# Three edits at the head of a fused attention and MLP kernel: an earlier gate, another PSUM bank, zeroed rows

## The chip, the cores and the metric

One core of a Trainium2 chip. The metric is the device time of one execution in microseconds, as the median of several.

## The reference

A gated linear attention, followed by two MLPs on its output. B=4, H=8, S=768, D=48.

```python
for t in range(S):                       # per batch and head
    cur = einsum('bhd,bhe->bhde', u * k[t], v[t])
    y[t] = einsum('bhd,bhde->bhe', r[t], state + cur)
    state = w[t][..., None] * state + einsum('bhd,bhe->bhde', k[t], v[t])
x = y.transpose(0, 2, 1, 3).reshape(3072, 384)
h = x @ w_in                             # 384 x 2048
x = (h * clip(h + 3, 0, 6) / 6) @ w_out  # 2048 x 384
out = ((x @ w1) * (x @ w2) @ w3) @ w_out2   # 384 x 1024, 1024 x 1024, 1024 x 384
```

All of it is float32.

## The kernel before

**Attention.** The 3072 tokens are cut into 12 groups (`p`) of 256, each of two chunks (`g` = 2p, 2p+1), each of two halves of 64 tokens. Arrays by row (`r_sb`, `k_sb`, `w_sb`) hold two heads: one in rows 0 to 47, one in rows 64 to 111. Rows 48 to 63 belong to no head. The tiles have 112 rows, and every VectorE operation on them and the transpose by TensorE go over all 112. The first of the two loads of each tile takes 64 rows of the source, so that rows 48 to 63 get finite values which are never used; the second takes 48 rows. Per group VectorE scales k and r by products of decays (`scale(p, n)`, n = 0 to 5), TensorE multiplies them at four levels (`level_products`), the products are merged into `A_own` (levels 0 and 1 by VectorE, levels 2 and 3 by ScalarE), and then come a transpose of k (TURN), the new states (STATES), and two steps READ_A and READ_B, each with a product of `A_own` and v (`read`) and one of state and r (`read_states`). `y_copy` then takes y out of PSUM. `scale(p, n)` for n of 2 or more waits for the products of level n-2. Four products by token per chunk, which need tokens loaded once more in another layout (`tok_a`, `tok_b`), are made by GpSimd and summed by VectorE (`sum_bands`); the load of the next such tokens waits for a sum.

**MLPs.** The first is cut into 96 slots of 128x512 hidden values: `hidden(n)` on TensorE, `clip(n)` on ScalarE, `gate(n)` on VectorE, then `split_gated(n)` (ScalarE) and `rest_of_gated(n)` (VectorE), which split the result into two fp32r parts, then `project(n)` on TensorE. Each matmul of float32 is three passes over such parts. The weights come in 16 pieces (0 to 7 of `w_in`, 8 to 15 of `w_out`), each loaded into a stage, rounded by ScalarE and its remainder formed by VectorE (both named `split_weight(q)`, L594 and L993). The stages are memory that `gated`, `g_hi` and `g_lo` use later; pieces 6 and 7 lie where `g_lo[0]` will be. Pieces 6 to 11 are issued by SyncE after the attention output has been moved into `x_sb`, piece q only when an earlier piece in its stage is split. `form_w34` forms w3 times w_out2 on TensorE; its 16 half steps stand between the attention steps of groups 0 and 1.

**Order.** Each engine's order is written out by hand for groups 0 and 1; from slot 0 on, a loop over the slots places the steps of the next groups among them. Before the first data TensorE runs eight matmuls of `y_sb`, twice recorded each, that compute nothing (`keep_busy`); they wait for the memset of `y_sb`. TensorE before: attention(1, 0), form_w34(4, 0), READ_B of group 0, form_w34(4, 1), its `read_states`, form_w34(5, 0), attention(1, 1), ... In `level_products`, level 1 of group 1 waits for `y_out` 2, since level 1 writes both banks of `ps_lv`, of which `y_bank` gives bank 1 to y. The loads of SyncE stand in the order of its `_` function: w, k, r of group 0, the first weights, tokens, v, w, k, r of group 1, and so on.

Of the kernel before, what the change touches and what calls it, by code (L numbers as in the profile page):

```python
# [11 lines left out]
B, H, S, D = 4, 8, 768, 48  # L12
# [4 lines left out]
HB = 64  # L17
# [84 lines left out]
def gated_linear_attention_two_mlps(nc, rT, kT, wT, r, k, v, w, u, w_in, w_out, w1, w2, w3T, w_out2,  # L102
# [3 lines left out]
    with ctx:  # L106
# [14 lines left out]
        def sem(name):  # L121
            return ctx.enter_context(nc.semaphore(name))
# [84 lines left out]
        y_zeroed = sem("y_zeroed")  # L207
        d_loaded = [sem(f"d_loaded{i}") for i in range(2)]
# [109 lines left out]
        def y_bank(half):  # L318

            return ps_lv[:, 1, :] if half else ps_att  # L320
# [38 lines left out]
        def _(sp):  # L359
            def load_by_row(dst, src, p, loaded):  # L360

                b, s0 = p * GT // S, p * GT % S
                for row, first, count in ((0, 0, HB), (HB, D, D)):
                    sp.dma_start(dst[row:row + count, :, :],  # L364
                                 src[first:first + count, b, :, s0:s0 + GT]
                                 ).then_inc(loaded[p % 2], 16)

            def load_w(p):
                load_by_row(w_sb, wT, p, d_loaded)

            def load_k(p):
                load_by_row(k_sb[p % 2], kT, p, d_loaded)

            def load_r(p):
                load_by_row(r_sb[p % 2], rT, p, r_loaded)
# [216 lines left out]
        def _(act):  # L592
# [33 lines left out]
            def y_copy(g):  # L626
                act.wait_ge(y_done, g + 1)
                if g >= 2:
                    act.wait_ge(x_moved[g % 2], CHUNK_X * (g // 2))
                y = y_sb[g % 2][:].rearrange("d a (half t) -> d half a t", t=SUB)  # L630
                of_half = [y_bank(half)[:, 0:PAIRS * SUB].rearrange("d (a t) -> d a t", t=SUB)
                           for half in range(2)]
                copy(y[:, 0], of_half[0][0:HP])
                for h in range(2):
                    last = copy(y[h * HB:h * HB + D, 1], of_half[1][y_row(1, h):y_row(1, h) + D])
                last.then_inc(y_out, 1)
# [101 lines left out]
            split_weight(3)  # L738
            store_w34(5)
            merge(1, 2)  # L740
# [4 lines left out]
            split_x(1)  # L745
            merge(1, 3)
            store_w34(7)
            split_weight(6)
            split_weight(7)
            act.wait_ge(three_made, 1)  # L750
            act.wait_ge(w_lo_done, 2)
            clip(0)
            split_weight(8)
# [58 lines left out]
        def _(dve):  # L812
# [203 lines left out]
            def rest_of_gated(n):  # L1016
                dve.wait_ge(g_hi_done, n + 1)
                if n >= 2:
                    dve.wait_ge(x2_part, n - 1)
# [3 lines left out]

            nc.vector.memset(three[:], 3.0).then_inc(three_made, 1)
# [30 lines left out]
            merge(1, 0)  # L1055
            split_weight(0)
            split_weight(1)
            scale(1, 3)
            merge(1, 1)
            sum_bands(2)  # L1060
            split_weight(2)
            scale(1, 4)
            split_weight(3)
            sum_bands(3)
# [3 lines left out]
            scale(1, 5)  # L1068
            keep(4)
            start(2)  # L1070
            start(3)
            split_weight(5)
            split_weight(6)
            split_weight(7)
            gate(0)
# [40 lines left out]
        def _(pe):  # L1116
# [8 lines left out]
            def level_products(p, step):  # L1125
# [7 lines left out]
                elif p == 1 and step == 1:  # L1133
                    pe.wait_ge(y_out, 2)
# [53 lines left out]
            def read(g):  # L1188
# [8 lines left out]
                for a in range(PAIRS):  # L1197
                    for half in range(2):
                        rows = slice(half * SUB, (half + 1) * SUB)
                        for h in range(2):  # L1200
                            first, at_row = c * DM + (2 * a + h) * D, y_row(half, h)
                            last = nc.tensor.matmul(
                                y_bank(half)[at_row:at_row + D, y_cols(a)],
# [5 lines left out]
            def read_states(g):  # L1209
# [6 lines left out]
                for a in range(PAIRS):  # L1216
                    for n in taking:
                        at_col = cols_of(p, c, a).start + n % 2 * SUB
                        for h in range(2):
                            rows, at_row = slice(h * HB, h * HB + D), y_row(n % 2, h)  # L1220
                            last = nc.tensor.matmul(
                                y_bank(n % 2)[at_row:at_row + D, y_cols(a)], state[n % 4][rows, a, :],
# [34 lines left out]
            def project(n):  # L1257
# [4 lines left out]
                if i == 0 and t > 0:  # L1262
                    pe.wait_ge(x2_copied, t)
# [53 lines left out]
            attention(0, READ_B)  # L1317
            form_w34(4, 1)
            attention_rest(0, READ_B)
            form_w34(5, 0)  # L1320
            attention(1, 1)
            form_w34(5, 1)
            form_w34(6, 0)
            attention(1, 2)
            form_w34(6, 1)
            attention(1, 3)
# [114 lines left out]
```

## Time and profile before

| | us |
|---|---|
| median of 3 runs | 898.12 (897.38 to 900.26) |
| the profiled execution | 897.8 |
| its span, first to last instruction | 896.0 |
| TensorE matmul busy | 878.5 |
| VectorE busy | 531.1 |
| ScalarE busy | 327.5 |
| GpSimd busy | 220.9 |

The profile is of one execution. Times of rows count from the span's start. Busy time of TensorE is of overlapping matmuls, so a busy TensorE isn't one at its peak; an idle one is idle. "PEld" is its weight load, "SPq" a queue's issue of a transfer. L594, L814 and L993 are helper lines, used by many operations: the tile names tell them apart.

### The profile page before, as it was taken

How to read it: one execution, taken by the hardware profiler on the slowest of the kernel's cores; microseconds unless marked ns; L12 is line 12 of the kernel's file. 1: busy time of each engine (PE TensorE's matmuls, PEld its weight loads, DVE VectorE, ACT ScalarE, POOL GpSimd, SP SyncE). 2: the span in 40 equal slices, each digit the busy share in tenths (PEclk: the TensorE clock that was granted, in tenths of full speed). 3: DMA queues.
4: the chain of work that ended last, by engine and by line, in shares of the span. 5: the costliest groups of instructions: out<-in, count | busy, mean ns of one | idle time of the engine just before them, and what ended most of it. 6: DMA issues, size and time to landing. Idle time of an engine off the chain costs nothing.

```text
span 896.0 us, 23934 instructions
## 1 busy us (share of the span) xinstructions
PE 878.5 (98%) x10452; PEld 790.8 (88%) x10452; DVE 531.1 (59%) x765; ACT 327.5 (37%) x556; POOL 220.9 (25%) x200
## 2 busy tenths in 40 slices
PE   8989899999999999999999999999999999999998
PEld 4557899999999999999999999998888888888887
DVE  4888997788887878786878734633231222323121
ACT  0435453435353535343444444632221312222212
POOL 0374245445444544444535000000000000000000
PEclk9998999999999999999999999999999999999999
DMA  9987653525252525353443102530010202010001
GB/s 289 339 262 240 203 136 105 155 89 162 82 161 81 160 83 159 92 150 99 144 129 92 37 21 79 181 112 1 12 60 1 71 0 71 1 36 1 25 11 36
DMA packets 62646, 93.31 MB, mean 104 GB/s; under 512 B 8215, under 2 KB 48622, under 8 KB 62542
## 3 DMA queue, kind: packets, MB, share of 16 engines
q1 hardware_dynamic: 59934, 88.36, 32.4%
q10 hardware_dynamic: 2608, 3.43, 1.3%
q8 instruction: 82, 1.34, 0.7%
q14 instruction: 22, 0.18, 0.1%
HBM read 76.03 MB, written 11.01 MB: 97 GB/s over the span
## 4 chain that ended last, share of the span: by engine, by line
PE 81%; DVE 8%; SPq 4%; DMA 3%; issue 2%; ACT 1%; ACTq 0%; DVEq 0%
PE ps_acc L1118 11%; PE ps_acc L1119 10%; PE ps_acc L1120 10%; PE ps_h L1118 10%; PE ps_h L1120 10%; PE ps_h L1119 10%; PE ps_lv L1119 4%; PE ps_lv L1120 4%; PE ps_lv L1118 4%; PE ps_lv L1152 3%; SPq L415 3%; DMA w3T_sb<-in_w3T 2%; DVE r_sb L814 1%; DVE k_sb L814 1%; SPq L364 1%
## 5 line engine op out<-in xcount | busy, mean ns | idle before, releaser
L550 POOL TENSOR_TENSOR tok_a<-tok_a 128x384 f32<-128x384 f32 x120 | 153.2, 1303 | 185.3 <-DMA tok_a<-in_k 185.3
L1118 PE MATMUL ps_acc<-g_hi,w_out_hi 128*128 128x256 f32 x576 | 169.9, 295 | 0.0
L1118 PE MATMUL ps_h<-x_hi,w_in_hi 128*128 128x256 f32 x576 | 165.3, 287 | 1.9 <-DVE gated L1012 1.9
L1119 PE MATMUL ps_h<-x_hi,w_in_lo 128*128 128x256 f32 x576 | 162.5, 282 | 0.0
L1120 PE MATMUL ps_h<-x_lo,w_in_hi 128*128 128x256 f32 x576 | 162.2, 282 | 0.0
L1119 PE MATMUL ps_acc<-g_hi,w_out_lo 128*128 128x256 f32 x576 | 162.0, 281 | 0.0
L1120 PE MATMUL ps_acc<-g_lo,w_out_hi 128*128 128x256 f32 x576 | 161.5, 280 | 0.0
L594 ACT ACTIVATE g_hi<-gated 128x512 fp32r<-128x512 f32 x144 | 90.9, 632 | 166.7 <-DVE gated L1100 107.8
L1100 DVE TENSOR_TENSOR gated<-gated,ps_lv 128x512 f32<-128x512 f32 x48 | 33.1, 689 | 186.3 <-PE ps_lv L1120 186.3
L1118 PEld LDWEIGHTS ps_h<-x_hi,w_in_hi 128*128 128x128 f32 x576 | 109.2, 190 | 4.1 <-DVE w_in_lo L993 2.0
L1118 PEld LDWEIGHTS ps_acc<-g_hi,w_out_hi 128*128 128x128 f32 x576 | 108.4, 188 | 4.0
L1119 PEld LDWEIGHTS ps_h<-x_hi,w_in_lo 128*128 128x128 f32 x576 | 109.3, 190 | 0.1
L1120 PEld LDWEIGHTS ps_h<-x_lo,w_in_hi 128*128 128x128 f32 x576 | 109.3, 190 | 0.0
L1120 PEld LDWEIGHTS ps_acc<-g_lo,w_out_hi 128*128 128x128 f32 x576 | 108.7, 189 | 0.0
L1119 PEld LDWEIGHTS ps_acc<-g_hi,w_out_lo 128*128 128x128 f32 x576 | 108.4, 188 | 0.0
L1020 DVE TENSOR_TENSOR g_lo<-gated,g_hi 128x512 fp32r<-128x512 f32 x96 | 76.0, 792 | 44.1 <-ACT g_hi L594 44.1
L692 ACT ACTIVATE gated<-ps_h,three 128x512 f32<-128x512 f32 x96 | 65.9, 686 | 71.4 <-PE ps_h L1120 71.3
L1012 DVE SCALAR_TENSOR_TENSOR gated<-gated,ps_h 128x512 f32<-128x512 f32 x96 | 65.6, 683 | 36.2 <-ACT gated L692 36.2
L594 ACT ACTIVATE gated<-ps_h 128x512 f32<-128x512 f32 x48 | 28.7, 598 | 109.8 <-PE ps_h L1120 109.8
L1120 PE MATMUL ps_acc<-w_lo,g_hi 128*128 128x384 f32 x192 | 64.6, 336 | 0.0
L1119 PE MATMUL ps_acc<-w_hi,g_lo 128*128 128x384 f32 x192 | 64.4, 336 | 0.0
L1118 PE MATMUL ps_acc<-w_hi,g_hi 128*128 128x384 f32 x192 | 64.3, 335 | 0.0
(97 smaller groups left out, 1541.5 us busy)
## 6 DMA issues: line engine op xcount, KB each, us to landing
tok_a<-in_r SPq DMA_DIRECT2D x21, 768.0 KB
tok_a<-in_w SPq DMA_DIRECT2D x21, 384.0 KB
v_sb<-in_v SPq DMA_DIRECT2D x12, 384.0 KB, 3.7
x_scratch<-x_out SPq DMA_DIRECT2D x12, 384.0 KB, 4.3
x_in<-x_scratch SPq DMA_DIRECT2D x6, 768.0 KB, 5.7
tok_a<-in_k SPq DMA_DIRECT2D x22, 192.0 KB
out<-x_out SPq DMA_DIRECT2D x5, 768.0 KB, 4.0
x_sb<-y_sb SPq DMA_DIRECT2D x144, 24.0 KB, 1.8
```

Of the source, the lines that this page charges most:

```text
L415: sp.dma_start(x_sb[g % 2][row % P:row % P + n, row // P, :], y_sb[g % 2][at_row:at_row + n, head // 2, :]).then_inc(x_moved[g % 2], 16)
L550: return nc.gpsimd.tensor_tensor(dst, x, y, ALU.mult)
L594: return nc.scalar.activation(dst, src, ACT.Copy, **scale)
L692: nc.scalar.activation(gated[n % 2][:], ps_h[n % 2][:], ACT.Relu, bias=three[:]).then_inc(relu_done, 1)
L814: return nc.vector.tensor_tensor(dst, x, y, ALU.mult)
L1012: nc.vector.scalar_tensor_tensor(out=gated[n % 2][:], in0=gated[n % 2][:], scalar=6.0, in1=ps_h[n % 2][:], op0=ALU.min, op1=ALU.mult).then ...
L1020: nc.vector.tensor_tensor(g_lo[n % 2][:], gated[n % 2][:], g_hi[n % 2][:].bitcast(F32), ALU.subtract).then_inc(g_lo_done, 1)
L1100: nc.vector.tensor_tensor(gated[n % 2][:], gated[n % 2][:], ps_lv[:, n % 2, :], ALU.mult).then_inc(ab_made, 1)
L1118: nc.tensor.matmul(psum, hi, moving_hi, start=start, stop=False)
L1119: nc.tensor.matmul(psum, lo, moving_hi, start=False, stop=False)
L1120: return nc.tensor.matmul(psum, hi, moving_lo, start=False, stop=stop)
L1152: last = nc.tensor.matmul(psum[s0:s0 + count, h, first:first + SUB // 2] .rearrange("s (n l) -> s n l", l=size), k_g[rows, s:s + count], of_r,
```

## The change

Three edits.

1. `y_bank(p, half)`: for group 0, half 1 of y goes to bank 2 of `ps_acc`, no longer to bank 1 of `ps_lv`. Hence level 1 of group 1 has no wait for `y_out`, and `project(0)` gets one (it writes `ps_acc`). TensorE runs levels 1, 2 and 3 of group 1 earlier by one to three half steps of `form_w34`; VectorE runs `scale(1, 3)` and `merge(1, 1)` ahead of the first two remainders of `w_in`, and its later scalings earlier too. `sum_bands(3)` and the splits of x come after `scale(1, 5)`.
2. `gate(0)` on VectorE stands ahead of the remainders of pieces 6 and 7, and `clip(0)` on ScalarE ahead of their roundings. `rest_of_gated(0)` waits for the remainders, whose stages it writes.
3. Rows 48 to 63 are no longer loaded. VectorE writes zeros to rows 32 to 63 of five tiles by five memsets, ahead of its other two memsets; the loads of rows 0 to 47 of groups 0 and 1 wait for them and come after those of rows 64 to 111.

```diff
-        def y_bank(half):
-            return ps_lv[:, 1, :] if half else ps_att
+        def y_bank(p, half):
+            if half == 0:
+                return ps_att
+            return ps_lv[:, 1, :] if p else ps_acc[:, KT - 1, :]
...
-                for row, first, count in ((0, 0, HB), (HB, D, D)):
-                    sp.dma_start(dst[row:row + count, :, :],
-                                 src[first:first + count, b, :, s0:s0 + GT]
+                for h in (1, 0):
+                    if h == 0 and p < 2:
+                        sp.wait_ge(rows_zeroed, zeroed_at)
+                    sp.dma_start(dst[h * HB:h * HB + D, :, :],
+                                 src[h * D:(h + 1) * D, b, :, s0:s0 + GT]
                                  ).then_inc(loaded[p % 2], 16)
...  ScalarE
             split_weight(3)
+            merge(1, 2)
             store_w34(5)
-            merge(1, 2)
             split_weight(4)
             store_w34(6)
             split_weight(5)
             split_x(0)
             split_x(1)
+            store_w34(7)
             merge(1, 3)
-            store_w34(7)
-            split_weight(6)
-            split_weight(7)
             act.wait_ge(three_made, 1)
             act.wait_ge(w_lo_done, 2)
             clip(0)
+            split_weight(6)
+            split_weight(7)
             split_weight(8)
...  VectorE
             def rest_of_gated(n):
                 dve.wait_ge(g_hi_done, n + 1)
+                if n == 0:
+                    dve.wait_ge(w_lo_done, NP)
...
+            for unused in (w_sb, k_sb[0], r_sb[0], k_sb[1], r_sb[1]):
+                nc.vector.memset(unused[HB // 2:HB, :, :], 0.0).then_inc(rows_zeroed, 1)
             nc.vector.memset(three[:], 3.0).then_inc(three_made, 1)
             nc.vector.memset(y_sb[0][:], 0.0).then_inc(y_zeroed, 1)
...
             merge(1, 0)
+            scale(1, 3)
+            merge(1, 1)
             split_weight(0)
             split_weight(1)
-            scale(1, 3)
-            merge(1, 1)
+            scale(1, 4)
             sum_bands(2)
             split_weight(2)
-            scale(1, 4)
             split_weight(3)
+            scale(1, 5)
+            keep(4)
             sum_bands(3)
             split_x(0)
             split_x(1)
             split_weight(4)
-            scale(1, 5)
-            keep(4)
             start(2)
             start(3)
             split_weight(5)
+            gate(0)
             split_weight(6)
             split_weight(7)
-            gate(0)
             split_weight(8)
...  TensorE
-                elif p == 1 and step == 1:
-                    pe.wait_ge(y_out, 2)
...  project(n)
-                if i == 0 and t > 0:
+                if n == 0:
+                    pe.wait_ge(y_out, 2)
+                elif i == 0:
                     pe.wait_ge(x2_copied, t)
...
             attention(0, READ_B)
+            attention(1, 1)
             form_w34(4, 1)
             attention_rest(0, READ_B)
             form_w34(5, 0)
-            attention(1, 1)
+            attention(1, 2)
             form_w34(5, 1)
+            attention(1, 3)
             form_w34(6, 0)
-            attention(1, 2)
             form_w34(6, 1)
-            attention(1, 3)
             form_w34(7, 0)
             form_w34(7, 1)
```

## Rows read from the trace of the kernel before

**Rows 1.** The page: span and busy times of the engines.
```profile
span 896.0 us, 23934 instructions
PE 878.5 (98%) x10452; PEld 790.8 (88%) x10452; DVE 531.1 (59%) x765; ACT 327.5 (37%) x556; POOL 220.9 (25%) x200
```

**Rows 2.** Windows: length, busy time (count) by engine, TensorE's granted clock, DMA share, GB/s.
```profile
73.00:75.00 2.00, 2.00 (x12) 1.47 (x11) 2.00 (x6) 0.18 (x1) 0.16 (x1) 1.00 1.06 398
...
140.00:160.00 20.00, 20.00 (x356) 19.04 (x355) 16.39 (x22) 6.79 (x13) 11.37 (x12) 1.00 0.27 89
```

**Rows 3.** The chain that ended last, in order of time: start, us, what.
```profile
77.82 3.05 DVE w_in_lo L993 x2
...
121.85 0.61 DVE r_sb L814
122.51 0.76 PE ps_lv L1152 x50
```

**Rows 4.** Who waited for whom, VectorE, 40 to 135 us: total, times, longest.
```profile
DVE totals L814 <- PE ps_lv L1152: 3.4, 1, 3.4
DVE w_in_lo L993 <- ACT w_in_hi L594: 2.3, 1, 2.3
```

**Rows 5.** Timeline, 0 to 13 us: start, us, engine, line, what [idle before].
```profile
0.81 0.06 DVE L1024 MEMSET three<- 128x1 f32 x1 [0.81 <-PEq L1430]
0.86 0.96 POOL L545 MEMSET A_own<- 128x1024 f32 x1
0.95 0.48 DVE L1025 MEMSET y_sb<- 112x512 f32 x1
1.49 6.32 PE L1278 MATMUL ps_acc<-y_sb 112*128 112x512 f32 x8 [1.49 <-DVE y_sb L1025]
7.64 1.88 PE L1278 MATMUL ps_lv<-y_sb 112*128 112x512 f32 x4
12.05 1.08 PE L1152 MATMUL ps_acc<-r_sb,k_sb 48*60 48x32 f32 x64 [0.81 <-DVE r_sb L814]
```

**Rows 6.** Timeline of TensorE, 43 to 74 us.
```profile
43.41 1.08 PE L1152 MATMUL ps_acc<-r_sb,k_sb 48*60 48x32 f32 x64 [1.03 <-DVE r_sb L814]
45.11 2.85 PE L1289 MATMUL ps_h<-w_out_sb,w3T_sb 128*128 128x384 f32 x8 [0.62 <-DMA w3T_sb<-in_w3T]
66.63 0.76 PE L1152 MATMUL ps_lv<-r_sb,k_sb 48*32 48x32 f32 x64 [1.98 <-DVE r_sb L814]
73.98 0.57 PE L1118 MATMUL ps_h<-x_hi,w_in_hi 128*128 128x256 f32 x1
```

**Rows 7.** Timeline of VectorE and GpSimd, 34 to 58 us.
```profile
34.36 4.78 POOL L550 TENSOR_TENSOR tok_b<-tok_b 128x384 f32<-128x384 f32 x4
35.37 1.51 DVE L814 TENSOR_TENSOR totals<-w_sb 112x512 f32<-112x512 f32 x1 [0.85 <-DMA k_sb<-in_kT]
...
48.95 2.67 POOL L550 TENSOR_TENSOR tok_a<-tok_a 128x384 f32<-128x384 f32 x2 [9.80 <-DMA tok_a<-in_k]
49.32 3.11 DVE L993 TENSOR_TENSOR w_in_lo<-w_stage,w_in_hi 128x768 fp32r<-128x768 f32 x2
56.17 1.50 DVE L814 TENSOR_TENSOR k_sb<-k_sb,totals 112x512 f32<-112x512 f32 x1
```

**Rows 8.** Timeline of VectorE, 74 to 84 us.
```profile
74.60 0.95 DVE L993 TENSOR_TENSOR w_in_lo<-w_stage,w_in_hi 128x768 fp32r<-128x768 f32 x1
80.79 0.67 DVE L1012 SCALAR_TENSOR_TENSOR gated<-gated,ps_h 128x512 f32<-128x512 f32 x1
82.47 1.49 DVE L1020 TENSOR_TENSOR g_lo<-gated,g_hi 128x512 fp32r<-128x512 f32 x1
```

**Rows 9.** Timeline of ScalarE, 74 to 79 us: pieces 6 and 7 of w_in.
```profile
76.93 1.59 ACT L594 ACTIVATE w_in_hi<-w_stage 128x768 fp32r<-128x768 f32 x2 [0.40 <-DMA w_stage<-in_w_in]
```

**Rows 10.** Timeline of SyncE's queue, 45 to 69 us.
```profile
45.05 0.33 SPq L385 DMA_DIRECT2D tok_b<-in_r  x1
67.88 1.06 SPq L404 DMA_DIRECT2D w_stage<-in_w_in  x2
```

More of the change, by code:

```diff
@@ L207, in gated_linear_attention_two_mlps @@
         y_zeroed = sem("y_zeroed")
+        rows_zeroed = sem("rows_zeroed")
         d_loaded = [sem(f"d_loaded{i}") for i in range(2)]
@@ L359, in _, with load_by_row @@
         def _(sp):
-            def load_by_row(dst, src, p, loaded):
+            def load_by_row(dst, src, p, loaded, zeroed_at):
                 b, s0 = p * GT // S, p * GT % S
-                for row, first, count in ((0, 0, HB), (HB, D, D)):
-                    sp.dma_start(dst[row:row + count, :, :],
-                                 src[first:first + count, b, :, s0:s0 + GT]
+                for h in (1, 0):
[3 more added lines that the diff above has]
+                                 src[h * D:(h + 1) * D, b, :, s0:s0 + GT]
                                  ).then_inc(loaded[p % 2], 16)
             def load_w(p):
-                load_by_row(w_sb, wT, p, d_loaded)
+                load_by_row(w_sb, wT, p, d_loaded, 1)
             def load_k(p):
-                load_by_row(k_sb[p % 2], kT, p, d_loaded)
+                load_by_row(k_sb[p % 2], kT, p, d_loaded, 2 + 2 * (p % 2))
             def load_r(p):
-                load_by_row(r_sb[p % 2], rT, p, r_loaded)
+                load_by_row(r_sb[p % 2], rT, p, r_loaded, 3 + 2 * (p % 2))
             def load_tok(g):
@@ L630, in y_copy @@
                 y = y_sb[g % 2][:].rearrange("d a (half t) -> d half a t", t=SUB)
-                of_half = [y_bank(half)[:, 0:PAIRS * SUB].rearrange("d (a t) -> d a t", t=SUB)
+                of_half = [y_bank(g // 2, half)[:, 0:PAIRS * SUB].rearrange("d (a t) -> d a t", t=SUB)
                            for half in range(2)]
@@ L1202, in read @@
                             last = nc.tensor.matmul(
-                                y_bank(half)[at_row:at_row + D, y_cols(a)],
+                                y_bank(p, half)[at_row:at_row + D, y_cols(a)],
                                 v_sb[rows, first:first + D], A_own[rows, h, c, a, :],
@@ L1221, in read_states @@
                             last = nc.tensor.matmul(
-                                y_bank(n % 2)[at_row:at_row + D, y_cols(a)], state[n % 4][rows, a, :],
+                                y_bank(p, n % 2)[at_row:at_row + D, y_cols(a)], state[n % 4][rows, a, :],
                                 flat(r_sb[p % 2])[rows, at_col:at_col + SUB],
```

## The prediction

> **What bounds the kernel now.** I read the busy times and the windows first, then the chain that ended last, then the waits of VectorE, then the timelines of the places that these name. TensorE is busy 878.5 of 896.0 us [rows 1], and in a window such as that from 140 us it has no idle time while VectorE has 3.6 us in 20 [rows 2]: there the kernel is paced by TensorE, and nothing in this change touches it. The chain shows another picture of the head. From about 55 us to 121.85 it runs through VectorE nearly all the way; the last piece of it is a scaling, 0.61 us from 121.85, which lets TensorE start a level product at 122.51 [rows 3]. So the end moves by as much as VectorE's list moves at that handover. On that list VectorE has, from 40 us on, two waits of over 0.5 us ahead of the handover: 3.4 us for level 1 of group 1 and 2.3 us for piece 6 of w_in [rows 4]. So at most 5.7 us can be had, 0.6% of the time, and the question is whether the time that is won at the first wait is kept at the second. Before 45 us the chain isn't VectorE's: a load of w3T holds TensorE until 45.11 [rows 6].
>
> **Edit 1, the bank.** Level 1 of group 1 no longer waits for y and comes right behind READ_B's first part. With nothing else changed, VectorE would find its products at about 49.5, have 0.2 us of wait for them where it had 3.4, and run ahead by some 3 us. The order of the rest costs nothing by itself: the same operations, and GpSimd's product pass from 48.95 lies beside whichever stands there. A scaling pass of 512 columns takes 1.50 us beside it [rows 7], and 0.6 on the chain where GpSimd is idle [rows 3]; the two remainders that change places with it are slowed likewise (3.11 us for two [rows 7], 0.95 for one without GpSimd [rows 8]). I price this exchange at 0, with 0.8 us to either side, one pass caught or missed.
>
> **Edit 3, at the start.** Five memsets of 1024 columns now stand ahead of that of y_sb on VectorE's queue, and TensorE's dummy matmuls wait for y_sb. The memset of 512 columns takes 0.48 us and that of one column 0.06 [rows 5]: 0.82 ns for each further column, 0.90 us for 1024, 4.5 us for five. Bounds: 2.4 us if 1024 columns cost no more than 512 (5 x 0.48), 4.8 us by GpSimd's memset of 1024 columns (5 x 0.96) [rows 5]. So the dummies start at 6.0 and not at 1.49.
>
> The Trainium skill (VectorE: DVE Perf Modes, "Zero memsets can be issued as uint32") says that a memset takes one cycle per element; at the 0.96 GHz it gives for VectorE that would be 1.07 us each, an estimate of 5.3 us for five, and 0.8 us more of late start. The row of 512 columns speaks against it slightly: by the rule it would take 0.53 us, the trace has 0.48.
>
> The dummies are 16 records. Eight take 6.32 us, the next four 1.88 [rows 5]: the first run at the lower of TensorE's two clock levels (0.86 us each, 1.2 GHz), and the change to 0.43 us each (2.4 GHz) comes some 5.2 us after the first. All of them take from 1.49 to 11.24, 9.7 us, and the first level product then waits 0.81 us for VectorE and starts at 12.05 [rows 5]. If the clock rises as long after the start as before, the dummies end at 6.0 + 9.7 = 15.7, less the overlap of the last two, and the level product starts at about 15.5: 3.5 us late. If it rose at the same moment as before, it would be 1.3 us; if 1.5 us later, with the dearest memsets, 5 us. I take 3.5, because the rise follows work.
>
> The wait for memsets in SyncE's queue: the first load of rows 0 to 47 waits from 1.4 to about 1.8 us and the next ones less. The loads and issues behind them come 0.3 us later, and each is 14% smaller (96 rows for 112). k_sb lands at 8.2, which TensorE, busy until 15.5, doesn't see. What is saved up to 45 us is six loads of 16 rows of 4 KB, 0.39 MB, at the 398 GB/s of a full DMA stream [rows 2] 1.0 us: w3T lands at about 44.
>
> **Where the late start goes.** TensorE runs without a gap from 12.05 to 42.38. Then it has two waits: 1.03 us for a scaling until 43.41 and 0.62 us for w3T until 45.11 [rows 6]. A scaling 1.1 us later (below) and w3T 1 us earlier leave both covered: TensorE uses 1.65 us of slack and is 3.5 - 1.65 = 1.85 us late at READ_B, 49.7 for 47.89. What is late next is VectorE: update(0) waits for the states, 3.5 us late, so scale(1, 0) starts at 37.9 for 35.37; GpSimd ends its pass at 39.1 (34.36 + 4.78) [rows 7], so two of the three operations cost 0.6 for 1.5 us, and VectorE is 1.1 us late at sum_bands(1). On that sum waits SyncE's queue: the token loads at 45.05 [rows 10] come 1.1 us late and with them all 20 transfers of x and everything behind them.
>
> **The list from 50 us, with both.** READ_B's first part ends at 50.3; merge(1, 0) to 51.2; level 1 at 50.3 to 51.4; scale(1, 3) beside GpSimd 3.3 us, to 54.7; merge(1, 1) 0.6; two remainders 2.7; VectorE is at 58.0, where before it had done the same by 59.6 (56.17, two passes of 1.50 and a merge of 0.6, less overlaps [rows 7]). That is 1.6 us ahead, what is left of 3.4 after 1.85. Level 2 comes at 57.5 (three half steps of 2.75 us behind 51.4 less the reads), its scaling at 58.6 to 61.8, sum_bands(2) 2.7, remainders 2 and 3 2.2, scale(1, 5) 1.4, keep 0.3, sum_bands(3) 2.4, x 0.9, piece 4 0.9, start 1.4, piece 5 0.9: 74.9 for 75.5 [rows 8].
>
> **Edit 2, the gate.** gate(0) (0.67 us [rows 8]) needs hidden(0). TensorE now has four half steps of w34 behind level 3, at 62.5: 4 x 2.75 = 11.0, so hidden(0) runs from 73.5 to 75.9 (before: a gap of 1.98 us, level 3 from 66.63, and only two half steps, which took until 73.98, 6.6 us, longer than 5.5 as they ran partly at the lower clock [rows 6]). clip(0) ends at 76.7, gate(0) at 77.3. It lies in what is still VectorE's wait for piece 6 and takes 0.6 us off the list behind it. Piece 6: its rounding starts at 76.93, held by the transfer [rows 9], which was issued at 67.88 [rows 10] into a stream that is full (398 GB/s from 73 to 75 us [rows 2]). The issue is 1.1 us later; k and r of group 2 are 0.13 MB smaller, 0.35 us. It lands at 76.9 + 1.1 - 0.35 = 77.7, or up to 0.4 us sooner, as piece 8 is issued later. The remainder of piece 6 then starts at 78.3, 0.5 us later than before (77.82 [rows 3]), behind its rounding of 0.8 (1.59 us for two [rows 9]). Pieces 6 and 7 take 3.05 [rows 3], piece 8 1.1: rest_of_gated(0) starts at 82.4 for 82.47 [rows 8]. Sum: +0.5 (piece 6) - 0.6 (the gate moved) = -0.1 us. The added waits cost nothing: y_out 2 is signalled at about 56, w_lo_done 8 one operation ahead on the same engine. From 82.5 to 122.4 VectorE has no wait and its list is the same, so this shift arrives. TensorE's wait of 1.9 us before slot 2 vanishes, but TensorE isn't what ends last there; nor do smaller loads later matter, with the DMA share at 0.27 [rows 2].
>
> 897.8 - 0.1 = 897.7 for the profiled execution; the median of the runs shown is 0.3 above it: 898.0.
>
> **The rivals.** (a) Part of it is kept. If the start costs 1.3 us only, TensorE's slack takes all of it, SyncE isn't late, piece 6 lands at 76.5, its remainder starts at 77.4 and the gate is out of the way: -0.4 - 0.6 = -1.0, 897.1. For it: the clock could rise at a time that isn't tied to the first dummy. Against: the row that shows 5.2 us. Chance 0.22. (b) Faster beyond the measurement. If piece 6 is there when VectorE asks for it, at 75.5 less what is gained, the whole of both waits is had: its remainder at 75.0, the gate behind it hidden, -2.8 to -3.5 us, 895.0. For it: 0.5 MB fewer bytes ahead of it and piece 8 no longer beside it. Against: the stream is full [rows 2] and 0.13 MB is 0.35 us of it. Chance 0.12. (c) The late start is felt in part. 5 us at the start leave 3.4 at READ_B and 2.6 on SyncE's queue; piece 6's remainder at 79.8: +2.0 - 0.6 = +1.4, 899.4. Chance 0.16. (d) Slower beyond it: the late start reaches SyncE's queue whole, since update(0), 3.5 to 5 us late, holds scale(1, 0) and GpSimd's pass still slows it. Then token loads, x moves and piece 6 are 3.5 to 4 us late, the remainder of piece 6 starts at 81.3, +3.5 - 0.6 = +2.9: 901.0. It decides from where sum_bands(1) is over 3.6 us late. Against: GpSimd's pass ends at 39.1, and VectorE had 0.85 us of wait there for k [rows 7]. Chance 0.08. (e) The change doesn't do what it says: level 1 comes no sooner than now, as y's other bank is held. Nothing on bank 2 of ps_acc is waited for after the merge of level 2 of group 0, so I put this under (c).
>
> **How the numbers follow.** The forecast, 898.0, has 0.42. A difference of 0.3%, 2.7 us, is about what a measurement of this kernel tells from none; the forecast, (a) and (c) lie within it. Same 0.80, faster 0.12, slower 0.08. The range leaves out the tails of (b) and (d): from 895.8, between (a) and (b), to 900.2, between (c) and (d).
>
> **What would show it.** In the new profile: the dummies starting near 6.0 and the first level product near 15.5 (edit 3 priced right); waits of TensorE at 42 to 45 us gone; level 1 of group 1 near 50.3, and no wait of 3.4 us on VectorE; SyncE's token loads near 46; piece 6's rounding held by its transfer at 77.3 to 77.7, with gate(0) ahead of it; rest_of_gated(0) near 82.4; the last VectorE hold on TensorE near 122.4. It is wrong if TensorE's start isn't late, if piece 6 lands before 76 or after 79, or if VectorE gets a wait between 82 and 122.

## The result, and the profile after

The changed kernel takes 908.02 us (906.78 to 909.24, 4 runs) where the kernel before takes 898.59 (897.38 to 900.26, 4 runs): ratio 1.0099, interval 1.0084 to 1.0115. It is slower by 9.4 us; the forecast was 898.0, no change. The profiled execution took 906.78 us with a span of 905.0, against 897.8 and 896.0 before [rows 1].

The page after, span and busy times, to read beside [rows 1]:

```profile
span 905.0 us, 23940 instructions
...
PE 878.6 (97%) x10452; PEld 792.2 (88%) x10452; DVE 541.7 (60%) x770; ACT 328.1 (36%) x556; POOL 223.4 (25%) x200
```

TensorE's busy time is the same to 0.1 us, so the 9 us are idle time of TensorE. VectorE's is 10.6 us more; five memsets of 0.91 explain 4.6 of them. The rest is other operations that took longer.

The timeline of VectorE after, from 0 to 7 us, answers to [rows 5]:

```profile
1.01 0.91 DVE L1032 MEMSET w_sb<- 32x1024 f32 x1 [1.01 <-PEq L1439]
2.08 0.91 DVE L1032 MEMSET k_sb<- 32x1024 f32 x1 [0.16 <-issue]
...
6.39 0.48 DVE L1034 MEMSET y_sb<- 112x512 f32 x1
```

And that of TensorE:

```profile
6.93 6.22 PE L1287 MATMUL ps_acc<-y_sb 112*128 112x512 f32 x8 [6.93 <-DVE y_sb L1034]
12.99 1.88 PE L1287 MATMUL ps_lv<-y_sb 112*128 112x512 f32 x4
...
16.51 1.08 PE L1159 MATMUL ps_acc<-r_sb,k_sb 48*60 48x32 f32 x64
```

Each memset has a busy time of 0.91 us, as forecast, but the next starts 1.07 us after it. The dummies start 5.44 us later than before and the first level product 4.46 later (12.05 to 16.51), since the wait of 0.81 us before it is gone and the dummies took 0.1 less (16.58 - 6.93 for 11.24 - 1.49).

The timeline of VectorE after, from 44 us, a stretch of which the prediction said that the order of the rest costs nothing:

```profile
48.21 2.08 DVE L911 COPY_PREDICATED A_own<-diag,corner 128x256 f32<-128x256 uint8 x2
50.19 1.15 DVE L958 TENSOR_TENSOR state<-kept,added 112x192 f32<-112x192 f32 x1
51.26 1.08 DVE L819 TENSOR_TENSOR totals<-totals 112x128 f32<-112x128 f32 x1
52.26 1.48 DVE L819 TENSOR_TENSOR k_sb<-k_sb,totals 112x512 f32<-112x512 f32 x1
53.66 1.48 DVE L819 TENSOR_TENSOR r_sb<-r_sb,totals 112x512 f32<-112x512 f32 x1
55.06 0.69 DVE L931 COPY_PREDICATED A_own<-lmask,ps_acc 124x512 f32<-124x512 uint8 x1
```

The same operations in the kernel before, VectorE, from 45.88 us:

```profile
45.88 0.78 DVE L906 COPY_PREDICATED A_own<-diag,corner 128x256 f32<-128x256 uint8 x2
46.56 0.35 DVE L953 TENSOR_TENSOR state<-kept,added 112x192 f32<-112x192 f32 x1
46.83 0.28 DVE L814 TENSOR_TENSOR totals<-totals 112x128 f32<-112x128 f32 x1
47.03 0.68 DVE L814 TENSOR_TENSOR k_sb<-k_sb,totals 112x512 f32<-112x512 f32 x1
47.63 0.68 DVE L814 TENSOR_TENSOR r_sb<-r_sb,totals 112x512 f32<-112x512 f32 x1
```

GpSimd after, the pass for chunk 2, which began at 48.95 before [rows 7]:

```profile
47.85 2.14 POOL L555 TENSOR_TENSOR tok_a<-tok_a 128x384 f32<-128x384 f32 x2 [8.02 <-DMA tok_a<-in_k]
```

Before, start(1), update(3) and scale(1, 2), the first five rows of each list, were done at 48.31, 0.64 us ahead of the pass. After, they come 2.33 us later and the pass 1.1 us sooner; start(1) begins 0.36 us behind the start of the pass, and all five rows lie in it (its last row ends at 56.0). They take 6.93 us, start of the first to end of the last, where they took 2.43: 4.5 us more. merge(1, 0), the sixth row, takes 0.69 us in the pass as it did outside; its data come from PSUM (`ps_acc`).

Who waited for that is seen in the timeline of TensorE after, from 43 us (before: [rows 6]):

```profile
43.48 2.85 PE L1298 MATMUL ps_h<-w_out_sb,w3T_sb 128*128 128x384 f32 x8
...
50.47 0.67 PE L1209 MATMUL ps_acc<-A_own,v_sb 64*48 64x64 f32 x32
55.89 1.34 PE L1159 MATMUL ps_lv<-r_sb,k_sb 48*56 48x32 f32 x64 [4.76 <-DVE A_own L931]
57.16 4.15 PE L1298 MATMUL ps_h<-w_out_sb,w3T_sb 128*128 128x384 f32 x8
61.24 0.67 PE L1228 MATMUL ps_acc<-r_sb,state 48*48 48x64 f32 x32
```

The two waits of before at 42 to 45 us are gone. But level 1 of group 1 waits 4.76 us, for merge(1, 0) (L931). The diff takes away the branch of p = 1 and step = 1, so level 1 falls into the general one below it:

```python
                elif step > 0:
                    pe.wait_ge(merged[p % 2], level(p, step - 1))
```

A wait for merge(1, 0) has thus taken the place of the wait for y_out. It is only the last part of the 4.76 us: level 1 also waits for scale(1, 2), which ends at 55.14, 4.0 us after TensorE was free (51.14); merge(1, 0) ends 0.6 us after that. Behind level 1 on TensorE stand form_w34(4, 1), which takes 4.15 us for 2.85 (the granted clock is 0.60 from 56 to 58 us and 0.54 from 58 to 60, so most of it ran at the lower of the two levels, 1.2 GHz; the engine had stood idle for the 4.76 us before), and then the second part of READ_B, `read_states`, at 61.24. Before, it came at 51.26. It gives y, which ScalarE copies (y_copy(1), 62.24 for 52.29), and y goes through SyncE's queue, which waits 6.8 us for it; in the list of its waits before there is none for y. SyncE after (before: [rows 10]):

```profile
49.69 20.49 SPq L420 DMA_DIRECT2D x_sb<-y_sb  x20
...
74.31 0.99 SPq L409 DMA_DIRECT2D w_stage<-in_w_in  x2
```

Pieces 6 and 7 are issued at 74.31 for 67.88. VectorE after, where they are used (before: [rows 8]):

```profile
82.80 0.69 DVE L1017 SCALAR_TENSOR_TENSOR gated<-gated,ps_h 128x512 f32<-128x512 f32 x1 [2.10 <-ACT gated L697]
85.27 2.68 DVE L998 TENSOR_TENSOR w_in_lo<-w_stage,w_in_hi 128x768 fp32r<-128x768 f32 x2 [1.78 <-ACT w_in_hi L599]
...
89.55 1.48 DVE L1027 TENSOR_TENSOR g_lo<-gated,g_hi 128x512 fp32r<-128x512 f32 x1
```

The chain that ended last, after (before: [rows 3]):

```profile
55.14 0.62 DVE A_own L931
55.89 1.34 PE ps_lv L1159 x63
57.23 4.09 PE ps_h L1298 x8
...
66.52 1.11 SPq L420
...
74.86 10.59 DMA w_stage<-in_w_in
85.47 0.86 ACT w_in_hi L599
86.35 1.60 DVE w_in_lo L998
...
130.31 0.76 PE ps_lv L1159 x50
```

rest_of_gated(0) is 7.1 us late (89.55 for 82.47) and the level product that the chain hangs on is 7.8 us late (130.31 for 122.51). The last 1.2 of the span's 9.0 us come later; this section doesn't place them.

### The profile page after: what moved, and what is told of

Same layout as the page of the kernel before. It is cut to its first block, busy times and chain, and to the rows that moved or that the text cites. A ratio compares the mean times of both kernels' runs of the same rounds, so it can differ in the third digit from the quotient of the medians.

```text
span 905.0 us, 23940 instructions
## 1 busy us (share of the span) xinstructions
PE 878.6 (97%) x10452; PEld 792.2 (88%) x10452; DVE 541.7 (60%) x770; ACT 328.1 (36%) x556; POOL 223.4 (25%) x200
## 4 chain that ended last, share of the span: by engine, by line
PE 78%; DVE 9%; SPq 6%; issue 3%; DMA 2%; ACT 1%; DVEq 0%; ACTq 0%
PE ps_acc L1127 11%; PE ps_acc L1128 9%; PE ps_acc L1129 9%; PE ps_h L1127 9%; PE ps_h L1129 9%; PE ps_h L1128 9%; SPq L420 5%; PE ps_lv L1128 4%; PE ps_lv L1129 4%; PE ps_lv L1127 4%; PE ps_lv L1159 3%; PE ps_h L1298 2%; DVE k_sb L819 2%; DVE r_sb L819 2%; DMA w_stage<-in_w_in 1%
## 5 line engine op out<-in xcount | busy, mean ns | idle before, releaser
L555 POOL TENSOR_TENSOR tok_a<-tok_a 128x384 f32<-128x384 f32 x120 | 150.6, 1282 | 192.7 <-DMA tok_a<-in_k 192.7
```

Of the source, the lines that this page charges most:

```text
L555: return nc.gpsimd.tensor_tensor(dst, x, y, ALU.mult)
```

## The experiments

The kernel before, run beside the experiments, took 899.41 us (31 runs) for the first four in the order of the text, 898.54 (28) for the next four, and 899.46 (35) for the last four. By the ratios the loss of the changed kernel is 8.9 us. Each kernel of the table ran ten times, but the changed one four, "y ahead of level 1" seven and the last two twelve times; each profile is of one execution, whose time is given where it isn't near the median. The expectations name theories by letter. **A**: the late start (edit 3) pushes VectorE's start(1), update(3) and scale(1, 2) into GpSimd's pass for chunk 2, and edit 1 has put y behind level 1, which waits for them. The rivals: **B**, the new order costs by itself; **C**, edit 3 costs by itself; **D**, it is the smaller loads or their waits; **E**, the contention acts through VectorE's list, and not through y being held; **F**, the pass isn't what slows VectorE; **G**, the added wait for merge(1, 0) is most of the loss; **H**, whatever is gained before 77 us ends in the wait for piece 6.

| kernel | median (lowest to highest) | ratio to before, interval |
|---|---|---|
| changed kernel | 908.02 (906.78 to 909.24) | 1.0099, 1.0084 to 1.0115 |
| edit 1 alone | 898.78 (897.14 to 901.02) | 0.9996, 0.9984 to 1.0009 |
| edit 2 alone | 900.28 (898.84 to 901.82) | 1.0007, 0.9994 to 1.0019 |
| edit 3 alone | 900.68 (899.14 to 902.31) | 1.0015, 1.0004 to 1.0026 |
| edits 1 and 2 | 899.80 (897.70 to 904.43) | 1.0007, 0.9988 to 1.0025 |
| y_sb's memset first | 898.30 (897.03 to 900.35) | 0.9993, 0.9980 to 1.0006 |
| y_sb's memset third | 897.60 (896.45 to 900.21) | 0.9974, 0.9960 to 0.9988 |
| loads of before | 902.40 (898.01 to 908.07) | 1.0039, 1.0012 to 1.0066 |
| y ahead of level 1 | 903.20 (898.32 to 907.86) | 1.0050, 1.0022 to 1.0078 |
| GpSimd's pass held | 900.42 (899.05 to 901.61) | 1.0018, 1.0007 to 1.0029 |
| no wait for merge(1, 0) | 904.58 (899.85 to 907.19) | 1.0053, 1.0034 to 1.0072 |
| y_sb first, no such wait | 898.28 (896.70 to 899.41) | 0.9985, 0.9973 to 0.9997 |
| the same, pass held | 898.64 (897.46 to 900.66) | 0.9987, 0.9976 to 0.9999 |

**Edit 1 alone** is the kernel before with the first edit's parts of the diff.

```diff
-            return ps_lv[:, 1, :] if half else ps_att
+            return ps_lv[:, 1, :] if p else ps_acc[:, KT - 1, :]
```

> Edit 1 alone (y in another bank, the new places of level 1 to 3, the new order of VectorE's scalings). Theory A: the loss needs both edits. The late start of edit 3 (5.4 us at the first dummy matmul) moves scale(1, 2) on VectorE into GpSimd's pass; edit 1 puts level 1, which waits for scale(1, 2), ahead of read_states on TensorE, so that y, the x moves and piece 6 of w_in are held. Alone, with scale(1, 2) ended at 48.3 as in the kernel before, level 1 starts at 48.6 without a wait over 0.5 us: 895.5 to 898, ratio 0.997 to 1.000. Theory B, the new order costs by itself, whatever the start: TensorE waits 3 us or more at level 1 and the ratio is 1.004 or more. Theory C, edit 3 alone makes the whole loss: here 0.997 to 1.000 too.

0.9996. In its profile scale(1, 2) ends at 47.97, ahead of the pass (48.57), and level 1 waits 1.01 us for merge(1, 0) and comes at 49.19, 0.6 us later than A had expected. VectorE runs scale(1, 3) from 50.35 where it began at 55.80, and is done with it, merge(1, 1) and two remainders at 56.77 for 59.69: 2.9 us ahead. But the remainder of piece 5 starts at 73.86 for 74.60, so most of that is gone before the wait for piece 6. VectorE's waits from 48 to 74 us fell by 1.5 us only (0.38, 1.30 and a new one of 0.62 for level 2, where they were 0.40 and 3.37), and the same operations took about 1 us longer. At pieces 6 and 7 it waits 1.92 and 1.12 us where it waited 2.27, and rest_of_gated(0) starts at 81.95, 0.5 us sooner than before.

**Edit 2 alone** is the kernel before with gate(0) and clip(0) moved and rest_of_gated(0)'s wait.

```diff
+            gate(0)
             split_weight(6)
             split_weight(7)
-            gate(0)
```

> Edit 2 alone (gate(0) and clip(0) ahead of pieces 6 and 7). All theories: gate(0) goes into VectorE's wait for piece 6 and 0.6 us is won, 898.0, ratio 0.9985 to 1.000. If it is above 1.001, clip(0) ahead of the roundings holds piece 6.

1.0007: nothing that can be measured, neither the gain of 0.6 us nor a loss. The profiled execution (900.84) shows something else. TensorE's granted clock was 0.50 from 14 to 22 us, where it was 1.00 in the profile before, and the second level product came at 17.79 for 14.97. VectorE in this run:

```profile
48.49 0.78 DVE L906 COPY_PREDICATED A_own<-diag,corner 128x256 f32<-128x256 uint8 x2
49.16 1.16 DVE L953 TENSOR_TENSOR state<-kept,added 112x192 f32<-112x192 f32 x1
```

GpSimd's pass began at 49.05, and scale(1, 2) was done at 54.13. So the order of before meets the pass too when TensorE is late for another reason than the memsets, and that execution, in which level 1 stands behind y, had a span only 3.0 us longer than the profile before (899.0).

**Edit 3 alone** is the kernel before with the memsets, the smaller loads and their waits.

```diff
+            for unused in (w_sb, k_sb[0], r_sb[0], k_sb[1], r_sb[1]):
+                nc.vector.memset(unused[HB // 2:HB, :, :], 0.0).then_inc(rows_zeroed, 1)
```

> Edit 3 alone (five memsets, rows 48 to 63 not loaded). Theory A: scale(1, 2) is in GpSimd's pass here too and ends at about 55, but level 1 of group 1 stands behind read_states and form_w34(5, 0), so y isn't held: y_copy(1) by 56, piece 6 rounded by 79, and VectorE waits for level 1 until about 58.5 (55.8 before): +2 to +3.5 us, ratio 1.002 to 1.004. Theory B: +1 to +3, with the rest of the loss in edit 1. Theory C, edit 3 makes the whole loss: +8 to +10, ratio 1.009 or more.

1.0015, 1.3 us, a little under what A had expected, with the whole late start in it. scale(1, 2) falls into the pass here too. VectorE in this run, from 47.5 us:

```profile
47.53 0.79 DVE L909 COPY_PREDICATED A_own<-diag,corner 128x256 f32<-128x256 uint8 x2
48.22 1.16 DVE L956 TENSOR_TENSOR state<-kept,added 112x192 f32<-112x192 f32 x1
...
51.70 1.48 DVE L817 TENSOR_TENSOR r_sb<-r_sb,totals 112x512 f32<-112x512 f32 x1
```

From start(1) to the end of scale(1, 2) it is 5.65 us. But in this order y stands ahead of level 1: y_copy(1) starts at 54.25 (52.29 before), and rest_of_gated(0) at 83.02. Rival C falls: the edit alone is a seventh of the 8.9 us.

**Edits 1 and 2** leave out the third edit.

> Edits 1 and 2 without edit 3: the start as before. Theory A: 895 to 897.5, ratio 0.996 to 0.999, level 1 of group 1 at 48.6, y_copy(1) ended by 54, rest_of_gated(0) at 81.5 or sooner. Theory B: ratio 1.004 or more. Theory C: as A.

1.0007, where A had expected a gain (0.996 to 0.999). The three edits alone add up to 0.18%, and the three together cost 0.99%, so the loss is in what edit 3 does together with the other two. That it is edit 1 and not edit 2 wasn't run as a pair; the traces and the run with y ahead of level 1, below, say so. Rival B falls with this as the cause of the loss at the median.

The order of edit 1 isn't harmless, though. The profiled execution is the slowest of the ten (904.43; another took 904.26). In it start(1) to scale(1, 2) are undisturbed (46.27 to 48.71), and TensorE in this run has:

```profile
45.97 4.54 PE L1293 MATMUL ps_h<-w_out_sb,w3T_sb 128*128 128x384 f32 x8 [1.08 <-DMA w3T_sb<-in_w3T]
...
52.12 1.03 PE L1154 MATMUL ps_lv<-r_sb,k_sb 48*56 48x32 f32 x64 [1.01 <-DVE A_own L928]
```

After two waits of about 1 us the granted clock is 0.50 from 48 to 50 us and a half step takes 4.54 us for 2.85. y_copy(1) comes at 56.85 and rest_of_gated(0) at 86.05. So with level 1 ahead of y one execution lost some 5 us against the median of the kernel before with neither a memset nor the pass in it; by this profile a late TensorE did it.

**y_sb's memset first** is the changed kernel with the five memsets behind the other two; edit 3 is all there, but the dummies start at 1.48 us.

```diff
-            for unused in (w_sb, k_sb[0], r_sb[0], k_sb[1], r_sb[1]):
-                nc.vector.memset(unused[HB // 2:HB, :, :], 0.0).then_inc(rows_zeroed, 1)
             nc.vector.memset(three[:], 3.0).then_inc(three_made, 1)
             nc.vector.memset(y_sb[0][:], 0.0).then_inc(y_zeroed, 1)
+            for unused in (w_sb, k_sb[0], r_sb[0], k_sb[1], r_sb[1]):
+                nc.vector.memset(unused[HB // 2:HB, :, :], 0.0).then_inc(rows_zeroed, 1)
```

> The changed kernel with the memsets of three and y_sb ahead of the five zeroing ones: the dummy matmuls start at about 1.5 us again; the loads are the small ones and wait for the zeros 0.6 us longer. Theory A (a late start of TensorE moves scale(1, 2) into GpSimd's pass, and level 1 holds y behind it): scale(1, 2) ends by 49, level 1 starts by 50, y_copy(1) ends by 55, ratio to the kernel before 0.997 to 1.001. Theory D (the smaller loads with their waits, not TensorE's start, make the loss): ratio stays at 1.008 to 1.011.

0.9993: the whole loss goes with the order of two lines. In its profile start(1) comes at 45.67 and takes 0.78 us, scale(1, 2) ends at 48.0 and the pass starts at 47.90; level 1 waits 1.21 us and is at 48.87, rest_of_gated(0) at 81.25. D, as the whole cause, falls.

**Loads of before**: the changed kernel with rows 48 to 63 loaded again; memsets and waits as changed.

```diff
-                    sp.dma_start(dst[h * HB:h * HB + D, :, :],
-                                 src[h * D:(h + 1) * D, b, :, s0:s0 + GT]
+                    count = D if h else HB
+                    sp.dma_start(dst[h * HB:h * HB + count, :, :],
+                                 src[h * D:h * D + count, b, :, s0:s0 + GT]
```

> The changed kernel with its five memsets and waits, but rows 48 to 63 loaded as before (over the zeros). It computes the same. Theory A: the bytes have nothing to do with the loss; TensorE starts at 6.9 as in the changed kernel, ratio 1.007 to 1.012. Theory D: the ratio falls to 1.002 or less.

902.4 with a spread of 10 us, where the changed kernel's is 2.5 and that of y_sb first 3.3. The pass starts at 48.93, as before the change, and start(1) at 48.03. VectorE in this run:

```profile
48.03 0.79 DVE L912 COPY_PREDICATED A_own<-diag,corner 128x256 f32<-128x256 uint8 x2
...
48.97 1.10 DVE L820 TENSOR_TENSOR totals<-totals 112x128 f32<-112x128 f32 x1
50.00 1.48 DVE L820 TENSOR_TENSOR k_sb<-k_sb,totals 112x512 f32<-112x512 f32 x1
```

A had said that the bytes have nothing to do with it (1.007 or more), and that is refuted: loading less made it worse by some 5 us at the median. In the profiles (this one took 904.32) the tokens of chunk 2 land 1.1 us sooner with the small loads, and the pass catches start(1) and update(3) as well as the scaling: 6.93 us where it is 4.85 here. It isn't all of the loss, so D holds in part. This execution also had a half step of 5.10 us for 2.85 behind level 1, at a granted clock of 0.50.

**y ahead of level 1**: the changed kernel with TensorE's order of before at this place.

```diff
-            attention(1, 1)
             form_w34(4, 1)
             attention_rest(0, READ_B)
+            attention(1, 1)
```

> The changed kernel with level 1 of group 1 moved behind form_w34(4, 1) and read_states(1) on TensorE. The late start and the slow scale(1, 2) stay (it ends at 55). Theory A: y isn't held, y_copy(1) ends by 57 for 63.4, SyncE's moves of x take 14 us for 20.5, piece 6 is rounded at about 79 for 84.4, ratio 1.002 to 1.005. Theory E (the loss is the late start and the contention themselves, carried by VectorE's list, and not the hold on y): ratio 1.007 or more.

903.2, again with a wide spread. In the profile y_copy(1) is at 54.76, 7.5 us sooner than in the changed kernel, and SyncE's moves of x take 14.28 us for 20.49; so the hold on y is a real part. The ratio is at the upper end of A's range; its interval reaches into E's (1.007 or more) but stays under the changed kernel's, so the contention that is carried by VectorE's list may be the other part. This execution lost time elsewhere, too. VectorE in this run:

```profile
47.92 2.41 DVE L911 COPY_PREDICATED A_own<-diag,corner 128x256 f32<-128x256 uint8 x2
...
77.23 4.71 DVE L911 COPY_PREDICATED A_own<-diag,corner 128x256 f32<-128x256 uint8 x4
...
87.92 0.68 DVE L1027 TENSOR_TENSOR g_lo<-gated,g_hi 128x512 fp32r<-128x512 f32 x1
```

start(2) and start(3) meet the next pass of GpSimd, from 76.39, and take 4.71 us; in the changed kernel the same four took 1.46. rest_of_gated(0) is at 87.92, only 1.6 us better.

**GpSimd's pass held**: the changed kernel, in which GpSimd waits for scale(1, 2) before its pass for chunk 2. The late start, the smaller loads, the added wait and the hold on y all stay.

```diff
             for g in range(1, 4):
+                if g == 2:
+                    pool.wait_ge(scaled[1], stage(1, 2))
                 products_by_token(g)
```

> The changed kernel with GpSimd's pass for chunk 2 held until scale(1, 2) has ended. Theory A: start(1), update(3) and scale(1, 2) take 3.2 us for 6.9, scale(1, 2) ends at about 51.5 for 55.1, level 1 starts at 52 and y_copy(1) ends at about 60; GpSimd's passes end some 4 us later, which may hold sum_bands(3): ratio 1.004 to 1.007. Theory F (GpSimd's pass isn't what slows these operations; it is the loads or the late start): scale(1, 2) ends at 54 or later, ratio 1.008 or more.

1.0018: 1.6 us are left of 8.9. VectorE in this run:

```profile
47.53 0.79 DVE L913 COPY_PREDICATED A_own<-diag,corner 128x256 f32<-128x256 uint8 x2
48.20 0.35 DVE L960 TENSOR_TENSOR state<-kept,added 112x192 f32<-112x192 f32 x1
...
49.28 0.68 DVE L821 TENSOR_TENSOR r_sb<-r_sb,totals 112x512 f32<-112x512 f32 x1
50.75 0.70 DVE L933 COPY_PREDICATED A_own<-lmask,ps_acc 124x512 f32<-124x512 uint8 x1 [0.79 <-PE ps_acc L1211]
```

GpSimd in this run:

```profile
50.04 1.95 POOL L555 TENSOR_TENSOR tok_a<-tok_a 128x384 f32<-128x384 f32 x2 [10.88 <-DVE r_sb L821]
```

Every operation has its duration of before. start(1) is even earlier than in the changed kernel (47.53 for 48.21), so it isn't the hold alone that differs. Edit 3 alone has start(1) at the same 47.53, though, and with the pass beside it took 5.65 us to the end of scale(1, 2); here it is 2.43, and 6.93 in the changed kernel. The pass itself is 2.2 us later, which doesn't outweigh it. Level 1 is at 51.59 for 55.89, rest_of_gated(0) at 83.36. The ratio is even lower than A had expected (1.004 to 1.007), and y_copy(1) is at 56.33. Rival F falls: this is the strongest of the runs.

**No wait for merge(1, 0)**: the changed kernel without the wait that the removed branch uncovered. scale(1, 2) is still waited for.

```diff
+                elif p == 1 and step == 1:
+                    pass
                 elif p == 1 and step in (2, 3):
```

> The changed kernel, in which level 1 of group 1 has no wait for merge(1, 0) (the kernel before had none). scale(1, 2) still has to be done. Theory A (the added wait is not the loss by itself: start(1), update(3) and scale(1, 2) lie beside GpSimd's pass and end near 55): level 1 at 55.2 for 55.9, y_copy(1) 0.7 us earlier, the time 907.3, ratio to the kernel before 1.007 to 1.010, if start(1) comes behind GpSimd's start as in the profile after. Rival G (the added wait is what cost most of it): level 1 near 50.5 to 52, ratio 1.002 or less.

1.0053, between the two expectations, so neither A's 1.007 nor G's 1.002 came true. TensorE in this run (907.19, the slowest of its ten):

```profile
55.02 1.23 PE L1161 MATMUL ps_lv<-r_sb,k_sb 48*56 48x32 f32 x64 [4.18 <-DVE r_sb L819]
```

Level 1 waits for the scaling, as A said, and comes 0.9 us sooner; 0.6 us of that is merge(1, 0). But the ratio is 0.0046 lower than the changed kernel's, nearly half of the loss, and nine of the ten executions lie below the changed kernel's fastest. Why the added wait is worth that much isn't shown, since the profile is of the slowest.

**y_sb's memset third**, a dose between: the dummies start at 3.71 us.

```diff
             for unused in (w_sb, k_sb[0]):
                 nc.vector.memset(unused[HB // 2:HB, :, :], 0.0).then_inc(rows_zeroed, 1)
+            nc.vector.memset(three[:], 3.0).then_inc(three_made, 1)
+            nc.vector.memset(y_sb[0][:], 0.0).then_inc(y_zeroed, 1)
+            for unused in (r_sb[0], k_sb[1], r_sb[1]):
+                nc.vector.memset(unused[HB // 2:HB, :, :], 0.0).then_inc(rows_zeroed, 1)
```

> The changed kernel, with the memsets of three and y_sb behind the second of the five zeroing memsets, so that the dummies start near 3.7 us (6.9 after the change, 1.5 with y_sb first). It is a dose between the two. Theory A (TensorE has 1.65 us of slack before READ_B and start(1) must come before GpSimd's pass of chunk 2 at 47.85): dummies 2.2 us later, some 0.5 us of it felt at READ_B, start(1) near 46.5 and 0.79 us long, ratio 0.998 to 1.002. Rival C (a loss in proportion to the late start): 9.4 x 2.2 / 5.45 = 3.8 us, ratio 1.004.

0.9974. So with the start 0, 2.2 and 5.4 us late the ratio is 0.9993, 0.9974 and 1.0099: nothing up to 2.2 us and all of it behind, not a loss in proportion (1.004 was expected from that). Where between 2.2 and 5.4 it begins wasn't run. At 2.2 us TensorE's slack takes it all (level 0 of group 1 is at 43.03, for 43.41 before); start(1) is at 45.51, only the last scaling pass touches GpSimd's (46.80), and level 1 is at 49.50. It is even the fastest of all kernels here, by 2.3 us against the kernel before (interval 1.1 to 3.6), just under the bound of 0.3%. Whether it is faster than y_sb first isn't shown, as the two intervals overlap, and its profiled execution was its slowest (900.21).

**y_sb first and no wait for merge(1, 0)**: both things that the prediction missed are taken away.

> y_sb's memset first, and no wait of level 1 for merge(1, 0): the changed kernel with both things that the prediction missed taken away. Theory A: level 1 at 48.3 for 48.87, y_copy(1) 0.5 us earlier than with y_sb first alone, ratio 0.997 to 0.9995. Rival H (what is gained before 77 us ends in the wait for piece 6, so nothing is left): 0.9985 to 1.0005, no difference from y first alone.

0.9985; level 1 is at 48.38 for 48.87. The difference from y_sb first alone, 0.9993, is smaller than either interval, so H isn't excluded as to the time. Its mechanism isn't in this profile: VectorE has no wait for piece 6 there. It waits 1.21 us for clip(0), runs gate(0) at 75.76 and goes on with the remainders (76.50) at once.

**The same, with GpSimd's pass held**:

> As y_first_free, and GpSimd's pass for chunk 2 waits for scale(1, 2), which here ends at about 48.0, the time at which the pass starts anyway. Theory A: start(1), update(3) and scale(1, 2) undisturbed in every execution, the pass at most 0.3 us later, ratio 0.997 to 0.9995, with a smaller spread than without the wait. Rival H: as without it, 0.9985 to 1.0005.

0.9987, with a spread of 3.2 us for 2.7, where A had expected a smaller one: where scale(1, 2) is ahead of the pass anyway, holding the pass brings nothing that can be measured.

## Why the prediction was wrong

**What bounds the kernel** was right. The end does move with VectorE's list: rest_of_gated(0) +7.1, the level product +7.8, the span +9.0.

**Edit 1, the first step that failed**: "Level 1 of group 1 no longer waits for y and comes right behind READ_B's first part." It waits for merge(1, 0) and, before that, for scale(1, 2): 1.01 us with edit 1 alone and 4.76 in the changed kernel. The prediction took level 1's start from TensorE's order and never read which branch of the waits the step falls into once its own is gone. It also didn't name what stands behind level 1: form_w34(4, 1), `read_states`, y, x and piece 6. It forecast 50.3 for level 1, and it came at 55.89.

**Edit 1, the second and the larger**: "The order of the rest costs nothing by itself", at 0 with 0.8 us to either side. The prediction looked only at operations inside the pass that change places with each other. Those that had just escaped it, start(1), update(3) and scale(1, 2), done 0.64 us ahead of it, it let through at 1.1 us later without asking whether the pass would catch them. They took 4.5 us more. This is the term that was put at nothing: with the pass held, 7.3 of the 8.9 us are gone. For what the sentence was written for, the exchange of places, edit 1 alone shows about 1 us more for the same operations, just outside the 0.8; and of the "some 3 us" that edit 1 was to win, 2.9 were there at 56.8 us and 0.7 at 73.9.

**Edit 3, mis-sized**: 4.5 us for five memsets were 5.35 (5 x 1.07), the dummies started at 6.93 and not at 6.0, and the first level product at 16.51 and not at 15.5. The busy time of a row is not the distance to the next one on its engine; between these there are 0.16 us each. The dummies took 9.65 us for 9.75, so the clock rose as long after their start as before, as was forecast. That the first of them ran at the lower level is read from their durations alone; the granted clock is given as 1.00 there in both profiles. The Trainium skill (VectorE: DVE Perf Modes, "Zero memsets can be issued as uint32") gives one cycle per element, which made an estimate of 5.3 us; the distance of 1.07 us from one memset to the next agrees, the busy time of 0.91 doesn't, and I took the row against it.

**Where the late start goes**: the covered waits at 42 to 45 us are right. But VectorE was 2.3 us late at sum_bands(1) (45.59 for 43.27) and at start(1), not 1.1, and SyncE's token loads likewise (47.37 for 45.05). update(0) was 4.5 us late instead of 3.5; 2.6 of that were taken back in scale(1, 0), which no longer waited for k and met less of GpSimd's first pass, much as argued.

**The pass comes sooner.** The prediction credited smaller loads with 1.0 us at w3T and with nothing else. The same 1.1 us brought the tokens to GpSimd at 47.85 and so the pass onto start(1); with the loads of before they came at 48.93.

**The list from 50 us.** "Three half steps" between level 1 and level 2 are two in the diff, form_w34(4, 1) and (5, 0); the 57.5 was added up with two and is right as a sum.

**Edit 2** isn't contradicted: alone it makes no difference (1.0007), and the 0.6 us it was credited with are less than the runs can tell. Here gate(0) waited 2.10 us for clip(0), as all of slot 0 was late.

**The rivals.** (d), slower, had the right sign and a chance of 0.08. Its mechanism, a late sum_bands(1) on SyncE's queue, was not the one: the queue waited for y. Its turning point, 3.6 us late at sum_bands(1), was far off: 2.3 us were enough to lose 8.9, as what is lost in the pass and behind it is more than the lateness itself.

The rule that would have named the cause stands in the Trainium skill, SBUF — State Buffer, "Who interferes with whom": a VectorE instruction with two inputs in SBUF contends with a GpSimd instruction that reads SBUF, and whichever issues first holds the shared ports for the whole instruction. The traces agree for the scalings (0.68 and 1.48 us), and for the predicated copies, which read a mask and data: 0.79 us for two where the pass hasn't begun, 2.08 and 2.41 where it has; merge(1, 0), a predicated copy with its data in PSUM, took 0.69 in the pass. The trace of the kernel before had it too, at start(0), just behind the start of GpSimd's first pass:

```profile
31.18 2.38 DVE L906 COPY_PREDICATED A_own<-diag,corner 128x256 f32<-128x256 uint8 x2
```

It is the row that the prediction should have priced start(1) by, once it had moved it to within a microsecond of the pass.

**What stays open**: the last 1.2 us of the span; how the 8.9 us divide between the slowed operations, the hold on y and the lower clock behind the wait, since no run takes away one and leaves the others as they are; and why most executions without the wait for merge(1, 0) are faster than the changed kernel. In the three kernels of the widest spread (7 to 10 us) start(1) begins within 0.9 us of the pass, so a race for the first start would fit. But in the changed kernel and in edit 3 alone it does too, with spreads of 2.5 and 3.2 us, and edits 1 and 2 have a spread of 6.7 with start(1) 3.5 us ahead of the pass. A half step at the lower clock (4.15 to 5.10 us for 2.85) stands in some profiles and not in others; that would fit as well. No two executions of one kernel were compared.

## What to carry to other kernels

When a branch with a special wait is removed, read which wait the step gets instead, and list what is queued behind it. When work on one engine ends shortly ahead of a pass of another that slows it, write down that distance (0.64 us here): a delay larger than it, or an earlier load, can cost more than itself, above all where the slowed work holds a queue (1.3 us with y ahead of level 1, 8.9 with y behind it). And a memset that nobody needs yet goes behind the one that something waits for: that order alone was worth some 9 us.

## What was not expected of the hardware

A predicated copy of 128x256 beside GpSimd's products of tokens grew from 0.4 to over 1 us (two took 0.78 and 2.08); four of them took 1.46 us in one run and 4.71 in another. An update of 192 columns went from 0.35 to 1.15 us and a scaling pass of 512 from 0.68 to 1.48, 0.8 us each: the small operation suffers most for its size. Loading 96 rows of w, k and r where it had been 112 made the changed kernel slower: 902.4 us with the loads of before, 908.0 with the smaller ones. Five memsets of 0.91 us busy time follow each other every 1.07 us.
